# Attention scores of two heads in the two halves of TensorE's rows, in a fused attention and MLP kernel

## What is computed

```python
scores = scale * np.matmul(q, k.transpose(0, 1, 3, 2))
kth = np.partition(scores, -32, axis=-1)[..., -32:-31]
scores = np.where(scores >= kth, scores, -1e9)
attn = softmax(scores)                       # over the 32 that are left
x = np.matmul(attn, v)                       # heads side by side: (4, 576, 512)
gate = sigmoid(causal_conv5(x, conv_w))
x = (gate * (x @ w_val)) @ w_out
u = x + real(fft2(x))                        # over tokens and features
out = u + relu(layernorm(u) @ w_ch1) @ w_ch2
```

## Time and profile before

| | |
|---|---|
| median of three runs | 1087.59 us (1083.38 to 1087.86) |
| the profiled execution | 1088.74 us |
| its span in the trace | 1086.7 us |
| TensorE matmul, busy | 987.4 us, 91% |
| VectorE, busy | 829.1 us, 76% |
| ACT, busy | 633.4 us, 58% |
| POOL, busy | 377.7 us, 35% |

### The profile page before, as it was taken

One profiled execution on the slowest core, in us unless ns is written; L12 is line 12 of the kernel. 1 busy time (PEld: TensorE's weight loads), 2 busy tenths in 40 slices (PEclk: granted clock), 3 DMA queues, 4 the chain that ended last, 5 costly groups with the idle time before them and its releaser, 6 DMA issues.

```text
span 1086.7 us, 19607 instructions
## 1 busy us (share of the span) xinstructions
PE 987.4 (91%) x6624; PEld 810.0 (75%) x6624; DVE 829.1 (76%) x1809; ACT 633.4 (58%) x1397; POOL 377.7 (35%) x520
## 2 busy tenths in 40 slices
PE   4877766899989999899999999999889999999997
PEld 3556555786778888775988888776778887668896
DVE  7999999998998998969988887889989943120000
ACT  5777887655666766546676755656666661122211
POOL 2575554223333332224342323234432122243221
PEclk9987988899999999989999999999999999999999
DMA  8556657020568777200877665220676774239874
GB/s 246 169 167 208 222 196 242 24 73 22 169 216 266 274 270 270 92 22 13 311 259 247 211 214 196 77 62 23 206 263 236 263 249 148 78 121 356 297 247 150
DMA packets 81186, 200.35 MB, mean 184 GB/s; under 512 B 8384, under 2 KB 26560, under 8 KB 81088
## 3 DMA queue, kind: packets, MB, share of 16 engines
q1 hardware_dynamic: 80928, 198.81, 54.3%
q10 hardware_dynamic: 160, 0.30, 0.1%
HBM read 177.58 MB, written 21.50 MB: 183 GB/s over the span
## 4 chain that ended last, share of the span: by engine, by line
PE 66%; DVE 19%; issue 6%; ACT 4%; DMA 2%; POOL 1%; SPq 1%; DVEq 0%; ACTq 0%; POOLq 0%
PE p_m L659 17%; PE p_m L673 16%; PE p_m L546 14%; DVE rest L879 9%; DVE top L885 7%; PE p_t L535 6%; PE p_s L505 5%; PE p_t L519 5%; DMA w_st<-w_split 2%; DVE top L870 1%; PE p_t L539 1%; ACT pT L763 1%; PE p_m L598 1%; ACT prob L749 1%; PE p_m L644 1%
## 5 line engine op out<-in xcount | busy, mean ns | idle before, releaser
L885 DVE MAX8 top<-rest 128x8 f32<-128x576 f32 x432 | 304.3, 745 | 0.0
L1116 POOL TENSOR_TENSOR hid_lo<-hid,hid_hi 128x256 fp32r<-128x256 f32 (+1 forms) x128 | 105.0, 820 | 319.3 <-ACT hid_hi L822 319.3
L879 DVE MATCH_REPLACE8 rest<-top,rest 128x576 f32<-128x576 f32 x288 | 211.4, 741 | 0.0
L659 PE MATMUL p_m<-un_hi,w_st 128*128 128x256 f32 (+1 forms) x1024 | 166.4, 306 | 19.0 <-ACT hid_hi L822 7.4
L673 PE MATMUL p_m<-w_st,hid_hi 128*128 128x512 f32 x576 | 182.1, 397 | 0.7 <-POOL hid_lo L1116 0.7
L659 PEld LDWEIGHTS p_m<-un_hi,w_st 128*128 128x128 f32 x1024 | 143.4, 191 | 31.2 <-issue 20.9
L737 ACT ACTIVATE s_sb<-p_s 128x576 f32<-128x576 f32 x144 | 93.2, 647 | 105.0 <-PE p_s L505 104.7
L519 PE MATMUL p_t<-id_sb,prob 128*128 128x128 f32 x720 | 109.8, 286 | 29.2 <-ACT prob L755 29.2
L821 ACT ACTIVATE hid<-p_m 128x256 f32<-128x256 f32 (+1 forms) x128 | 51.3, 401 | 142.5 <-PE p_m L659 142.5
L505 PE MATMUL p_s<-k_hi,q_st 128*128 128x288 f32 x320 | 109.9, 359 | 18.3 <-ACT s_sb L737 9.1
L535 PE MATMUL p_t<-pT,v_sb 128*64 128x128 f32 (+1 forms) x1600 | 108.8, 287 | 19.4 <-ACT pT L763 19.4
(11 more groups left out here) (99 smaller groups left out, 1543.4 us busy)
## 6 DMA issues: line engine op xcount, KB each, us to landing
w_st<-w_split SPq DMA_DIRECT2D x256, 512.0 KB, 4.5
w_split<-w_st SPq DMA_DIRECT2D x32, 512.0 KB, 3.2
k_raw<-kT SPq DMA_DIRECT2D x62, 144.0 KB, 3.0
q_raw<-qT SPq DMA_DIRECT2D x60, 144.0 KB, 2.9
u<-w_ch SPq DMA_DIRECT2D x32, 256.0 KB, 4.0
v_sb<-v SPq DMA_DIRECT2D x16, 256.0 KB, 3.2
wslot<-w_val SPq DMA_DIRECT2D x4, 1024.0 KB, 7.6
wslot<-w_out SPq DMA_DIRECT2D x4, 1024.0 KB, 5.3
```

Of the source, the lines that this page charges most:

```text
L659: mm = pe.matmul(mbank(HIDDEN_BANK[g], n), w1_st[i % NB1][:, w, k, :], x[:, k, at:at + n], start=part + k == 0, stop=part + k == KC + 1)
L879: dve.match_replace(rest[tt % 2][:, :], top[tt % NK][:, 8 * n - 8:8 * n], src[:, :], LOWEST).then_inc(s_chain, 1)
L885: found = dve.max(top[tt % NK][:, 8 * n:8 * n + 8], rest[tt % 2][:, :])
```

## The change

Both heads of a pair share one set of buffers. Rows 0 to 63 hold head 0, rows 64 to 127 head 1, in `q_hi`, `q_lo`, `k_hi` and `k_lo`. A tile is now 128 queries of both heads against one half of the keys: tile 2j the first 288 keys, tile 2j + 1 the other 288. Its matmuls use 64 rows each, head 0 the upper half of the array and head 1 the lower, with their results in the two banks of `p_s`. Three terms are summed, hi*hi, lo*hi and hi*lo; lo*lo is left out. That is six matmuls of 288 columns for a tile. Tile 8 keeps matmuls of 128 rows: its 64 queries of head 0 and 64 of head 1 stand in different columns with zeros in the other head's rows, so a sum over all rows is the right one; it has six matmuls in place of eight.

The scores of a unit lie side by side in `s_all`, which holds four units. A search starts when both tiles of its unit have been copied. Queries and keys of both heads come in one load each (and two small ones for the last 64 queries), at slot 7 of a pair for the pair after next; `hi` of queries and keys is made at slots 0 and 2, `lo` at 1 and 3, one operation each.

```diff
-LOAD = {8: 0, 4: 1}
-HIGH_Q, HIGH_K, LOW_Q, LOW_K = {0: 0, 5: 1}, {1: 0, 6: 1}, {2: 0, 6: 1}, {3: 0, 7: 1}
+LOAD_AT = 7
+HIGH_Q, LOW_Q, HIGH_K, LOW_K = 0, 1, 2, 3
+HIGH_Q0, LOW_Q0, HIGH_K0, LOW_K0 = 2, 3, 4, 5
...
-        s_sb = [sb(f"s_sb{i}", [P, S]) for i in range(NS)]
+        s_all = sb("s_all", [P, NU, 2, S])
...
+                def load_keys(p):
+                    if p:
+                        sp.wait_ge(s_lo, 2 * p)
+                    b, p = divmod(p, PAIRS)
+                    sp.dma_start(k_raw[:, :], kT[b, 2 * p:2 * p + 2].rearrange("h d n -> (h d) n")).then_inc(s_k_in, 16)
+
+                def load_queries(p):
+                    sp.wait_ge(s_lo, 2 * p)
+                    n = p
+                    b, p = divmod(p, PAIRS)
+                    sp.dma_start(q_raw[:, 0:WHOLE],
+                                 qT[b, 2 * p:2 * p + 2, :, 0:WHOLE].rearrange("h d n -> (h d) n")).then_inc(s_q_in, 16)
+                    load_left_queries(n, sp)
...
-                    cols = slice(P * (i // 2), P * (i // 2) + P)
-                    for o in range(2):
-                        parts = [(h, k[h][p % 2]) for h in heads for k in (k_hi, k_lo)]
-                        for n, (h, k) in enumerate(parts):
-                            mm = pe.matmul(p_s[:, o, 0:HALF_S], q_st[h][p % 2][:, cols],
-                                           k[:, o * HALF_S:o * HALF_S + HALF_S], start=n == 0,
-                                           stop=n == len(parts) - 1)
+                    terms = [(q_hi[p % 2], k_hi[p % 2]), (q_lo[p % 2], k_hi[p % 2]), (q_hi[p % 2], k_lo[p % 2])]
+                    if i == TILES - 1:
+
+                        for o in range(2):
+                            for n, (q, k) in enumerate(terms):
+                                mm = pe.matmul(p_s[:, o, 0:HALF_S], q[:, WHOLE:QW], k[:, o * HALF_S:o * HALF_S + HALF_S],
+                                               start=n == 0, stop=n == 2)
+                    else:
+                        o, c0 = i % 2, P * (i // 2)
+                        for n, (q, k) in enumerate(terms):
+                            for h in range(2):
+                                at = slice(D * h, D * h + D)
+                                mm = pe.matmul(p_s[:, h, 0:HALF_S], q[at, c0:c0 + P],
+                                               k[at, o * HALF_S:o * HALF_S + HALF_S], start=n == 0, stop=n == 2)
                     mm.then_inc(s_qk, 1)
...
-                            dve.wait_ge(s_copy, tt + 1)
+                            dve.wait_ge(s_copy, copies_upto(tt))
...
+                def low_queries(p):
+                    pool.wait_ge(s_qhi, p + 1)
+                    pool.tensor_tensor(q_lo[p % 2][:, :], q_raw[:, :], q_hi[p % 2][:, :].bitcast(F32),
+                                       ALU.subtract).then_inc(s_lo, 1)
```

More of the change, by code:

```diff
@@ L20 @@
 TAPS = 5
-NS = 6
-FILLS = 18
+FILLS = 15
 TOPK = 32
@@ L42 @@
 XW = TAPS - 1 + S
+NU = 4
+WHOLE = (S // P) * P
+QW = WHOLE + P
 HALF, HALF_S = 256, S // 2
@@ L241, in build @@
         s_feat_ev = sem("s_feat_ev")
-        s_qk_in = [sem(f"s_qk_in{h}") for h in range(2)]
+        s_q_in = sem("s_q_in")
+        s_k_in = sem("s_k_in")
         s_v_in = [sem(f"s_v_in{i}") for i in range(2)]
-        s_hi = sem("s_hi")
-        s_lo = [sem(f"s_lo{h}") for h in range(2)]
+        s_qhi = sem("s_qhi")
+        s_khi = sem("s_khi")
+        s_lo = sem("s_lo")
         s_qk = sem("s_qk")
@@ L309, in due, with unit_tiles, scores_of, copies_upto @@
             return 0 <= s - lag < ALL_TILES
[L311 to L315, removed]
+        def unit_tiles(n):
+            p, j = divmod(n, 5)
+            return TILES * p + min(2 * j + 2, TILES)
+        def scores_of(t):
+            return s_all[:, unit_of(t) % NU, tile_of(t)[1] % 2, :]
+        def copies_upto(t):
+            return unit_tiles(unit_of(t))
         def split_at(s, first, others):
             p, i = divmod(s, TILES)
-            h = (others if p else first).get(i)
-            return (p + 1, h) if h is not None and p + 1 < ALL_PAIRS else None
+            return p + 1 if i == (others if p else first) and p + 1 < ALL_PAIRS else None
         def unit_due(s):
@@ L448, in step @@
                                     sp.dma_start(out[bb, c0:c0 + m, :], u_row(bb, r)).then_inc(m_put, 16)
-                for half in range(2):
-                    sp.dma_start(k_raw[D * half:D * half + D, :], kT[0, 0]).then_inc(s_qk_in[0], 16)
-                load_qk(0, 1)
+                load_keys(0)
+                sp.wait_ge(s_zero, 1)
+                load_left_queries(0, sp)
                 sp.wait_ge(s_zero, FILLS)
@@ L467, in _ @@
                     p, i = divmod(s, TILES)
-                    ahead = p + 2 - LOAD.get(i, 0)
-                    if i in LOAD and ahead < ALL_PAIRS:
-                        load_qk(ahead, LOAD[i])
+                    if i == LOAD_AT and p + 2 < ALL_PAIRS:
+                        load_queries(p + 2)
+                        load_keys(p + 2)
                     i = part_due(s, 1)
@@ L822, in step @@
                         act.activation(hid_hi[i % 2][:, 0:width(b, g)], bank, ACT.Relu).then_inc(m_hev, 1)
[L824 to L829 removed]
+                act.dma_start(q_raw[:, 0:WHOLE], qT[0, 0:2, :, 0:WHOLE].rearrange("h d n -> (h d) n")).then_inc(s_q_in, 16)
+                high_keys(0)
+                high_queries(0)
                 for s in plan:
```

147 lines of the change are left out of this document (50 added, 97 removed).

## The result

| | before | after |
|---|---|---|
| median | 1087.86 us, 7 runs (1083.38 to 1091.28) | 1094.84 us, 7 runs; 1094.1 us for the six of 1093.05 to 1095.2 |
| the profiled execution | 1088.74 us | 1094.84 us |
| its span | 1086.7 us | 1092.8 us |

The ratio is 1.0058, with a 95% interval of 1.0037 to 1.0079: slower by 0.6%. One of the seven executions after, of 1625.4 us, was disturbed and is left out of the ratio. The forecast was 1093.

The account below looks back on a forecast made before the run. VectorE was taken to set the pace until 205 us, TensorE from 205 to 905. Tiles and seams +10.6, queue -4.5, ACT and POOL -0.5, start -0.5 gave +5.1 on 1088.74: 1093.8, about 1093 as a median; range 1078 to 1117.

Parts of the forecast that it names:

- The bodies: TensorE's plain score tiles: six half-row matmuls run as three steps of 0.13 us, 0.13 us less per tile.
- The rival of halves one after another: TensorE's score matmuls: row halves don't run side by side, time 1116 or, fully in series, 1127; chance 0.2.
- The seams, per tile: TensorE around plain tiles: shape changes cost 0.20 entering, 0.15 leaving; net +0.22 us for 65 tiles, +0.02 for 31.
- 0.9 of it: TensorE's tile sum of +11.8 us, 205 to 905 us: VectorE-bound slots absorb part, leaving +10.6 us.
- The second rival: TensorE's idle 27 us, 205 to 905 us, hides seams: 1087 with half hidden, 1080 with all; chance 0.12.
- The closing tiles: TensorE, 12 tiles that close a pair: six whole-row matmuls for eight, -0.26 us each, -3.1 us in all.
- SyncE's queue: SyncE's w_st loads no longer late behind POOL's splits: 4.5 of 5.5 us back, bounds 0 and 5.5.
- ACT and POOL: Three copies and three subtractions fewer per pair, showing only at TensorE's ReLU waits: -0.5 us, bounds 0 and -3.
- The start: First scores and VectorE's first search: fewer loads and copies ahead, -0.5 us, bounds -1 and +1.
- The score buffers: VectorE's search waits for both tiles of a unit, with eight tiles buffered for six: no effect on time.
- for nothing before: Stretch before tile 36, paced by VectorE's search: the change to TensorE's time per tile counts for nothing there.

Follow-up runs that it names:

- one slot more of distance: Changed kernel with every stage behind the scores one slot later and five unit buffers for four; 1093.69 us, ratio 1.0057.
- the unit wait: Kernel before, with only VectorE's first search of a tile made to wait for the copies of its whole unit; 1086.89 us, ratio 1.0002.
- the filler: Kernel before, with matmuls whose results nobody reads added in slots 16 to 41; 1090.30 us, ratio 1.0009.
- whole rows: Changed kernel with four whole-row matmuls per plain tile for six in row halves (scores not the reference's); 1082.31 us, ratio 0.9949.
- late splits: Changed kernel with splits at slots 5, 6, 6 and 7 and loads of raw operands at slot 8; 1090.69 us, ratio 1.0021.

## Why the prediction was right in sum and wrong in two steps

- **The bodies: right.** Three steps of 0.13 us. The rival of halves one after another would show six even starts. The trace has pairs.
- **The seams, per tile: right** (+0.22 us, with 79 idle places of the loads for 33). That 0.9 of it would reach the end of the chain was wrong: the run without row halves gives 0.58, 8.6 us for 13.4. The second rival, seams that fall into waits, was there in part. I took the share from the chain's listing of VectorE (4.4%) alone. Six of the 65 tiles stand beside a stop of TensorE already, which the count left out; where the rest went is not shown, for TensorE's waits are as long with row halves as without (23.5 us and 23.2 us in the five longest of each list between 205 and 905 us).
- **The closing tiles: right** in their pitch. That 2.8 us of their 3.1 reach the end was not measured.
- **SyncE's queue: mis-sized.** 4.5 us was forecast with bounds 0 and 5.5, and 5.75 was measured by itself, in one trace. That is what TensorE's idle time at w_st had given, with nothing absorbed.
- **ACT and POOL: -0.5 forecast, nothing measured.**
- **The start: right up to tile 24** (-0.57 us).
- **"The score buffers: nothing ... I see no place where it would" failed**, and with it "for nothing before" in the first part. It is the largest error: 8.5 us in this trace, for tile 36. I read "VectorE busy 192.00 of 192" as proof that TensorE's time does not count there, and did not measure how much later its loop could be before VectorE noticed. The wait is harmless alone (1.0002). What the traces show is a loop of TensorE and ACT that became late. Two stops of VectorE for a copy of scores, 2.63 and 2.91 us, make its search of tile 36 5.2 us late. Any one of three remedies takes most of that away and leaves it between -0.8 and +0.6 us: no row halves, a higher clock, other slots of the splits. Their gains at tile 36 (4.8, 4.8 and 4.7 us) don't add up, since each removes the same two stops.
- **What is left open of it.** The exponents of tile 36 stay 2.6 to 3.8 us late with any of these remedies and 4.5 us with two of them. Only one slot more of distance took that away (-4.4), and it lost as much later. Which part of the change makes it is not shown.

With the measured terms, the stretch from tile 36 to 138 gives +8.6 - 2.8 - 5.75 = 0.05 us, for a measured -2.2; if the closing tiles reach the end by 0.58 as well, it gives +1.0. The remaining 2 to 3 us are open. They are no scatter of the changed kernel: five traces of its later stretch give -2.0 to -3.3. The kernel before is known there from fewer (0, -0.3 with the unit wait, +1.8 with the filler).

Also open is why the granted clock fell in the first stage. It is the same in both kernels up to 112 us:

| us | 50 to 85 | 85 to 112 | 112 to 135 | 135 to 160 | 160 to 205 |
|---|---|---|---|---|---|
| before | 0.87 | 0.73 | 0.93 | 0.80 | 0.81 |
| after | 0.85 | 0.73 | 0.73 | 0.70 | 0.71 |
| whole rows | 0.85 | 0.71 | 0.87 | 0.64 | 0.73 |
| late splits | 0.85 | 0.73 | 0.87 | 0.66 | 0.75 |

The shorter tile of three terms and the idle time at the seams can't be the whole reason: the run with whole rows has neither in its plain tiles, and its clock is as low from 135 us on.

So a total of 1093 for a measured 1094.84 hides two errors: +9.0 us up to tile 36 (+8.5 for -0.5) and -7.8 behind it (-2.2 for +5.6). That they nearly cancel was luck.

## What to carry to other kernels

An engine that is busy 100% of a stage says who is last, not how far behind the next one is. Before calling an edit free in such a stage, measure the slack of the loop that feeds the busy engine, at the clock of that stage, and ask what a wait for more of its input does to it.

Packing two half-height matmuls side by side works, but each change between whole rows and halves costs more than what leaving out the fourth term saves in a tile (0.13 us); by these figures (0.20 + 0.15 us for both seams) three such tiles would have to stand together before it pays, which no run tried. And look for the part of a change that can be had by itself: one more buffer for raw keys made the kernel 0.8% faster, where the whole of the change made it 0.6% slower.

## What the runs showed of the hardware

- Two 64-row fp32r matmuls of 288 columns in different row halves run at once, at the pitch of one whole-row matmul (0.13 us), and so do their loads. By the Trainium skill (TensorE: Matmul & The Clock Gate, Part 3: Packing small matmuls — row/col tiling), matmuls in different tiles of the array run at the same time; this trace agrees.
- A change between whole array and row halves costs some 0.09 to 0.10 us in which no matmul starts, and the first load of weights behind it is not hidden (0.11 us for 128 columns of scores, 0.05 for a transpose), at the 2.4 GHz level.
- 53 matmuls of 256 columns without a use raised the granted clock of a stage from 0.79 to 0.91 and made it 0.4% faster, in the changed kernel (the two intervals, from 1.0037 and up to 1.0039, just touch); in the kernel before the same rise (0.85 to 0.92) gave nothing.
